# A fused attention and two-layer expert kernel: both halves of the weighted v go one product further back in the third position of each stage

## What is computed

```python
k_p = k.reshape(B, H, Sp, 8, D).mean(axis=3)
v_p = v.reshape(B, H, Sp, 8, D).mean(axis=3)
attn = softmax(scale * q @ k_p.T)
x = attn @ v_p                     # 8 x 8 x 576 x 64 -> 4608 x 512
h = (x @ w1) * (x @ w2) @ w3
x = h @ w_out
e_idx = argmax(x @ w_gate + modality_bias[modality_id])
out[mask] = gate_w * (relu(x[mask] @ w1[e]) @ w2[e])
```

## Time and profile before

| | us |
|---|---|
| median of three runs | 1297.41 |
| lowest and highest | 1287.84, 1299.17 |
| the profiled execution, its own time | 1282.49 |
| its span | 1280.7 |
| TensorE busy in the span | 1184.3 (92%) |
| VectorE, GpSimd, ScalarE busy | 675.8, 556.6, 398.7 |

### The profile page before, as it was taken

The page is one execution under the profiler, slowest core; times in us unless marked ns, Lnnn a source line. Parts: engine busy times, 40 slices in busy tenths (PEclk is TensorE's granted clock), DMA queues, the critical chain, the costliest instruction groups (busy, mean ns, idle before and its releaser), DMA issues.

```text
span 1280.7 us, 29767 instructions
## 1 busy us (share of the span) xinstructions
PE 1184.3 (92%) x11982; PEld 1092.2 (85%) x11983; DVE 675.8 (53%) x1260; ACT 398.7 (31%) x906; POOL 556.6 (43%) x565
## 2 busy tenths in 40 slices
PE   9989999999999999999999996898878899878887
PEld 7778999999999999999999984777767789767776
DVE  1997988988888665344454742222223353223222
ACT  1665556555554323332222410111111131111111
POOL 2446777777675555100000144444443346433343
PEclk9999999999999999999999996888998999898998
DMA  9836446356363233444445422311111101111111
GB/s 351 299 109 185 129 122 198 114 150 189 92 179 93 84 96 117 155 132 141 125 139 177 147 57 86 123 42 37 39 35 33 33 26 53 37 33 33 33 42 42
DMA packets 103779, 137.88 MB, mean 108 GB/s; under 512 B 20083, under 2 KB 70003, under 8 KB 103668
## 3 DMA queue, kind: packets, MB, share of 16 engines
q1 hardware_dynamic: 41060, 79.51, 19.9%
q10 hardware_dynamic: 53040, 36.29, 9.7%
q0 software_dynamic: 9568, 20.51, 5.3%
HBM read 93.58 MB, written 43.21 MB: 107 GB/s over the span
## 4 chain that ended last, share of the span: by engine, by line
PE 45%; another core or an unknown queue 12%; issue 1%; ACT 1%; DVE 1%; DMA 1%; POOL 0%; ACTq 0%; POOLq 0%; DVEq 0%
PE rt L786 6%; PE rt L787 6%; PE rt L788 6%; PE x2p L786 5%; PE ab L788 5%; PE x2p L788 4%; PE ab L787 4%; PE ab L786 4%; PE x2p L787 4%; ACT hth L1403 1%; DVE htl L1977 1%; DMA g_rows<-gst 1%; PE ab L942 0%; POOL gst L667 0%
## 5 line engine op out<-in xcount | busy, mean ns | idle before, releaser
L1977 DVE SCALAR_TENSOR_TENSOR htl<-ab,hth 128x512 fp32r<-128x512 f32 x76 | 52.3, 691 | 282.0 <-ACT hth L1403 216.9
L787 PE MATMUL ab<-xtl,e1h 128*128 128x256 f32 x608 | 170.5, 280 | 1.6 <-issue 1.6
L786 PE MATMUL ab<-xth,e1h 128*128 128x256 f32 x608 | 169.7, 279 | 1.5 <-issue 1.5
L1403 ACT ACTIVATE hth<-ab 128x512 fp32r<-128x512 f32 x76 | 45.3, 597 | 401.2 <-PE ab L788 225.6
L788 PE MATMUL ab<-xth,e1l 128*128 128x256 f32 x608 | 169.3, 278 | 0.6 <-issue 0.4
L751 POOL DMA_INDIRECT xq<-x_rows,idx_q x152 | 144.9, 953 | 55.9 <-issue 42.1
L762 POOL DMA_INDIRECT out<-y_out,tok_c x38 | 38.6, 1016 | 228.5 <-DVE y_out L1998 224.9
L786 PE MATMUL x2p<-e2h,hth 128*128 128x512 f32 x152 | 70.1, 461 | 60.7 <-DVE htl L1977 55.4
L788 PEld LDWEIGHTS ab<-xth,e1l 128*128 128x128 f32 x608 | 114.2, 188 | 2.6 <-issue 2.6
L786 PEld LDWEIGHTS ab<-xth,e1h 128*128 128x128 f32 x608 | 114.1, 188 | 2.7 <-issue 2.1
L787 PEld LDWEIGHTS ab<-xtl,e1h 128*128 128x128 f32 x608 | 114.4, 188 | 1.2 <-issue 0.5
(11 more groups left out here) (236 smaller groups left out, 3523.6 us busy)
## 6 DMA issues: line engine op xcount, KB each, us to landing
gr<-g_rows SPq DMA_DIRECT2D x36, 512.0 KB, 3.7
kv<-in_v SPq DMA_DIRECT2D x24, 512.0 KB, 4.8
qt<-in_q ACTq DMA_DIRECT2D x38, 256.0 KB, 4.3
kv<-in_k SPq DMA_DIRECT2D x16, 576.0 KB, 5.2
g_rows<-gst ACTq DMA_DIRECT2D x72, 128.0 KB, 2.9
g_rows<-gst ACTq DMA_DIRECT2D x36, 256.0 KB, 3.3
x_rows<-xr SPq DMA_DIRECT2D x36, 256.0 KB, 2.2
stage<-in_moe_w SPq DMA_DIRECT2D x8, 1024.0 KB, 8.4
```

What stands on the lines that cost most here:

```text
L786: pe.matmul(outp, lh, rh, start=first, stop=False)
L787: pe.matmul(outp, lh, rl, start=False, stop=False)
L1403: act.activation(hth[:, 2 * n:2 * n + 2, :].rearrange("p f n -> p (f n)"), ab[n // 2][:, n % 2, :], ACT.Relu).then_inc(hth_ready, 1)
L1977: dve.scalar_tensor_tensor(out=htl[:, fs, :].rearrange("p f n -> p (f n)"), in0=ab[n // 2][:, n % 2, :], scalar=0.0, in1=hth[:, fs, :].rea ...
```

## The change

```diff
-                    if i == 2 and n == 2 and b + 1 < B:
+                    if i == 2 and n == 3 and b + 1 < B:
                         weigh_v(b + 1, 0)
-                    if i == 2 and n == 4 and b + 1 < B:
+                    if i == 2 and n == 5 and b + 1 < B:
                         weigh_v(b + 1, 1)
```

## The result

The changed kernel takes 1311.99 us (median of 4, 1309.03 to 1312.92), the kernel before 1292.7 in the same comparison: a ratio of 1.0148, 95% interval 1.0109 to 1.0187. That is 19.3 us slower (the interval is 14 to 24 us); 19.5 were forecast. The profiled execution of the changed kernel took 1312.92 us, 30 more than the one before. Of these 19.9 lie between the first product of stage 0 and the first matmul of the next part, which is what the change can touch. The rest lies behind it, above all in the expert phase, which also spreads between executions of one kernel: what follows the stages' products took 777.2 us in this profile of the changed kernel and 768.5 in a second one.

What follows compares the result with a forecast made beforehand. TensorE was taken to bound the products' stretch (busy 389.55 of 396.49 us), VectorE having the least to spare of the other engines. 21.9 - 2.4 = 19.5 us on the median 1297.4 gives 1316.9 us, range 1296 to 1324.

Steps and rivals of the forecast that it cites:

- the delay: Product 5 of the fourth position starts later: 3.3 us in each of six stages, 2.1 in stage 6, sum 21.9 us.
- what comes back: Product 0 of the third position, stages 1 to 6: its wait for VectorE shrinks by 0.4 us each, 2.4 in all.
- the two terms of the forecast: Loss of 21.9 us at product 5 of the fourth position, less 2.4 at product 0 of the third: 19.5.
- The bursts' own cost: On TensorE, seven stages: each burst still holds it 1.71 us and about 0.1 for neighbouring products, so 0 change.
- the first burst: Third position: product 3 now precedes this burst, which starts 1.42 us later; no wait for the shared bank, 0.
- The copies and the copy of product 5: ScalarE behind the second burst: copies start 1.42 us later, product 5's queues behind them, 0.5 us left before product 1: 0.
- Five turns in a row: Fourth position: GpSimd's pause goes, five VectorE operations are stretched instead of two, product 2 is taken at 234.96, not 231.66.
- A: Rival, chance 0.13: fourth position's last turn lost in all stages; 2.1 us each, 14.7 - 2.4 = 12.3 us, 1309.7.
- B: Rival, chance 0.13: VectorE let in back to back in the fourth position; not slower, 0.4 x 7 = 2.8 us, 1300.2.
- C: Rival, chance 0.07: slack takes all 1.42 us and two waits inside bursts go; -0.8 us, 1296.6.
- D: Rival, chance 0.05: ScalarE's copy of product 5 misses product 1 of the fourth position too; 3.5 us on top, 1320.4.
- What should show: Product 5 about 5.0 us behind product 4 (3.8 in stage 6), GpSimd without pause, third position's product 0 wait 0.1.

## Why the prediction was right

The forecast (+19.5 us, by turns of VectorE and GpSimd behind the second burst, paid at product 5 of the fourth position) held in its mechanism and its place. That its size came out right is luck: the delay was put 4.9 us too high, what comes back 3.2 too low, and the clock's 8.5 were not there at all. Without the clock's share the two terms of the forecast, as measured, give 11.4 us.

- The bursts' own cost, 0, and the first burst, 0: right in the products' stretch (run with the first alone).
- The copies and the copy of product 5 come 1.42 later, and there is no wait at product 1: right (ScalarE at 228.76 and 230.07, the second 0.2 to 0.3 earlier than in the replay).
- Five turns in a row: right, line by line. Product 5's delay by them: 3.3 a stage and 2.1 in stage 6 was too much. Measured 2.4 to 2.7 and 1.5, in all 17.0 instead of 21.9. In the replay each turn costs about 0.5 us on top of GpSimd's instruction. GpSimd's ends came 2.26, 1.70, 1.14 and 1.66 us apart, where the instructions alone take 1.85, 1.28, 0.73 and 1.28: 0.4 on top. The row also began 0.2 to 0.3 us earlier than replayed.
- What comes back: I took 2.4 with that as the bound; it was 5.2, and 0.4 more behind stage 6. The wait at product 0 of the third position went whole; with the slow start behind it, it was worth 3.4 us in six stages and not 2.4. About 1.6 of the 5.2 are two stops inside bursts ("issue"), which no other profile here repeats, not even those with TensorE's order unchanged, so they seem to belong to that one execution. The rest is small differences in both directions.
- The clock: not in the prediction at all. Behind all six stops of 2.5 to 2.8 us the granted clock fell, at a cost of 8.5 us in the first profile of the changed kernel.
- Rivals: A did not come, the last turn was there in all six stages; its price (a turn less: 2.1 instead of 3.3, so 1.2 us a stage) is what the run with v pooled later shows (3.05 instead of 4.29). B is out: GpSimd got in at every handover. C is out, D did not come.
- What should show: the 5.0 us between products 4 and 5 was 4.1 to 4.4 (3.2 instead of 3.8 in stage 6); the wait at product 0 is gone.
- The base: 1316.9 was given on a median before of 1297.4; in the comparison that median was 1292.7, and the changed kernel's is 1312.0.
- The earlier trace rows was read as the stretch of the nine stages' products; it ends early in the ninth. Over all nine TensorE is busy 423.35 of 431.20 us, and nothing in the sum hangs on it.

The "GPSIMD Engine Reference" page of the Trainium skill, Specifications, has GpSimd's way to SBUF shared with VectorE and in contention with VectorE's instructions that have two SBUF inputs. The trace agrees (0.68 us alone, 1.18 to 2.22 beside GpSimd), and it adds that the two alternate one instruction at a time, at about 1.2 us for the turn taken away here.

## What to carry to other kernels

An operation moved on the engine that sets the end can be free there and cost on the engines behind it: ask what waits in the queue behind whoever reads its result, and whether a pause closes there. Where VectorE and GpSimd both work on two SBUF operands, look at GpSimd's instructions that follow each other without a pause: here each let one VectorE operation through, at 1.14 to 2.26 us a turn instead of the 0.6 at which VectorE's operations follow each other alone, and a pause of 1.07 us in that row let two through unhindered. Put the take-out that frees a PSUM bank ahead of work that nobody waits for yet, but look which product needs the next one.

## What the runs showed of the hardware that I had not expected

The granted clock fell to 0.50 for about one product behind stops of TensorE of 2.5 to 3.0 us, and it did not do so each time: in six of six stages in one profile of the changed kernel, four of six in another, two of six with only the second burst moved. Each fall behind product 5 cost 1.3 to 1.6 us. Shorter stops can do it too: behind stops of 1.7 us it fell in stage 5 of the run with v pooled later and, at a wait for data (1.74 us), in stage 0 of the first run of the kernel before with product 2 earlier, but not in stage 6 of three profiles with stops of 1.66 to 1.69 us. Behind none of the stops of 0.6 to 1.5 us in the stages' products did it fall, nor at all there with the stop filled by 20 matmuls. What decides between two stops of one length is open.

The kernel before took 1292.7, 1289.8, 1159.2 and 1283.4 us in the four comparisons, a spread of a tenth that goes with the chip and not with the kernel. The two profiles of the version with product 2 earlier show where it lies: the stages' products take 430.0 and 426.7 us and the second layer 214 in both, but the experts take 428.0 us on the chip of the 1159.2, at a granted clock of 1.00, and 550.1 on the other, at 0.91 and with more waiting. The changed kernel's ratio came out at 1.0148 and 1.0146 in the two comparisons where it ran.
